# Local attention with a pooled branch and two expert layers: the order of the first two units, of one copy on ACT and of four weight loads

## The chip, the cores and the metric

One core of a Trainium2 chip runs the whole program. The metric is the device time of one execution in microseconds (us). Times inside an execution are counted from the first instruction of the profiled one. ACT is ScalarE, and the SP queue is the queue of loads that SyncE issues.

## What is computed

Per batch and head, attention over 576 positions in two branches that are added: a local one (keys at a distance under 4) and one in which queries, keys and values are averaged by fours, with its output repeated four times. Two layers with a nonlinearity between two products follow.

```
out_d = sm_attn(q_d, k_d, v_d)              # pooled by 4, 144 positions
out_up = np.repeat(out_d, 4, axis=2)
mask = np.abs(pos[:, None] - pos[None, :]) < 4
scores = np.where(mask, scale * q @ k.T, -1e9)
x = out_up + softmax(scores) @ v            # batch 4, heads 8, seq 576, head_dim 64
h = x @ w_in;  g = h * tanh(softplus(h));  x = g @ w_out      # 2304 x 512, d_ff 2048
h = x @ w_in2; s = h * softmax(h); x = layernorm(s) * g_ln @ w_out2   # d_ff 1024
```

## The kernel before

The attention stage works on 16 units (`UNITS`); a unit is one batch and two heads, whose 2 x 64 dimensions fill the 128 partitions. The order on each engine is written out by hand: each engine has one loop over u, and the engines meet at semaphores. Unit u is scored in step u and its output is made in step u + 2 (`LATE`).

What happens to a unit:

- SyncE loads queries and keys into `qkT` (three buffers, L406, L407), windows of V for the local branch into `vw` (four loads, L389), and V in rows of four positions into `v4` (`v` in the profile, L415, L417). Its loop over s issues queries and keys of unit s, windows of unit s - 3 and V of unit s - 2. In steps 14 and 15 it adds the first quarter of the first layer's w_in, two loads of 256 KB in each (`load_w_in(0, kdx)`, L395, into `wraw`). The other quarters and w_out follow behind the loop.
- GpSimd sums queries and keys by four (`pool_queries_keys`, L489, L491; VectorE does the keys of every second unit and both of unit 0, L1079) and the values (`pool_values`, L500, L501), and multiplies the local probabilities with the reciprocal of their sum (`normalise_local`, L508).
- TensorE makes the pooled scores (`score_pooled`, L590), then the local scores in ten windows with a mask added by a matmul (`score_local`, L603, L609). Two steps later it turns both sets of probabilities (`turn_pooled` L624, `turn_local` L633) and multiplies them with the values (`value_pooled` L644, `value_local` L660).
- VectorE takes the maxima of the pooled scores (`maxima_pooled`, L1104, L1107, giving `pbias`), then maximum and subtraction of the local ones (`subtract_local`, L1113, L1116), later the sum of the local exponentials (`sum_local`, L1123) and the reciprocals of all denominators at once (`denominators`, L1130, L1132), which wait for both branches. It copies the local output into `xy` (`evict_local`, L1140).
- ACT takes the exponentials (`exp_pooled` L843, with sums; `exp_local` L874), normalises the pooled probabilities (`normalise_pooled`, L852), copies the turned ones (L864, L869), and copies the pooled output into `od` (`evict_pooled`, L878).

Towards the end of the loops the first layer begins. A float32 weight or activation is split into a high part, rounded to the type that TensorE multiplies fast, and a low part, the rest. ACT makes high parts (`weights_in_high` L885, `split_x` L893), VectorE low ones (`weights_in_low` L1165, `split_x` L1160). `weights_in_high(f)` waits for all four loads of its quarter. On TensorE `hidden(0, 0)` to `hidden(0, 2)` (L674) stand between the last turns and outputs: the first behind the turn of unit 14, the second behind its values, the third behind the turn of unit 15. `turn_pooled(u)` waits for `od_ok` of unit u - 1, that is for `evict_pooled(u - 1)`, since both use one PSUM bank. From there on the first layer runs over 6 blocks of tokens and 16 pieces of d_ff, then the second layer over 18 blocks of tokens.

## Time and profile before

| what | value |
|---|---|
| time, median of 3 runs | 712.12 us (711.85 to 713.67) |
| profiled execution | 710.95 us |
| its span, first to last instruction | 709.2 us |
| busy: TensorE, VectorE, ACT, GpSimd | 679.5, 366.8, 261.1, 184.4 us |
| granted TensorE clock, mean | 0.998 |

The span is 1.75 us shorter than the profiled execution's time, and that time is 1.17 us below the median. GpSimd's 184.4 us lie for the most part in the attention stage. A busy TensorE is not a TensorE at its peak, since matmuls are pipelined.

### The profile page before, as it was taken

The page shows a single profiled execution, that of the slowest core. Times are in us where ns is not written, and L with a number is a line of the kernel's source. Part 1 is how long each engine was busy: PE and PEld are TensorE (multiplying, and loading weights), DVE is VectorE, ACT ScalarE, POOL GpSimd, SP SyncE. Part 2 cuts the span into 40 slices and gives each one's busy share as a digit, 9 for nine tenths or more (in the row PEclk, how much of TensorE's full clock was granted, in tenths as well). Part 3 has the DMA queues.
Part 4 walks back from the last instruction along what each step waited for, and adds up shares of the span by engine and source line. Part 5 has one row for each costly group of instructions (what it writes and reads, how often), then busy time and mean ns, then how long its engine had stood idle before and what let it go on. Part 6 is the DMA issues. An engine that isn't in the chain of part 4 may idle for free.

```text
span 709.2 us, 12611 instructions
## 1 busy us (share of the span) xinstructions
PE 679.5 (96%) x5098; PEld 630.8 (89%) x5098; DVE 366.8 (52%) x675; ACT 261.1 (37%) x583; POOL 184.4 (26%) x221
## 2 busy tenths in 40 slices
PE   5888789999999999999999999999989999999998
PEld 4777679999999999999999999999768888888886
DVE  6999867642233223322232322564796667656671
ACT  3888665332112211221121122135564544444441
POOL 4899830000000000000000000584535434354100
PEclk9999999999999999999999999999999999999999
DMA  6877784000000000000000030002100000000001
GB/s 212 233 228 233 225 275 179 1 0 1 1 1 1 0 1 1 1 1 0 1 1 1 1 118 1 1 1 68 53 16 16 30 31 16 16 31 30 31 16 44
DMA packets 25657, 37.51 MB, mean 53 GB/s; under 512 B 2944, under 2 KB 13184, under 8 KB 25472
## 3 DMA queue, kind: packets, MB, share of 16 engines
q1 hardware_dynamic: 25600, 36.72, 16.2%
q8 instruction: 40, 0.66, 0.4%
q14 instruction: 17, 0.14, 0.1%
HBM read 31.99 MB, written 4.72 MB: 52 GB/s over the span
## 4 chain that ended last, share of the span: by engine, by line
PE 83%; POOL 8%; issue 4%; DVE 3%; DMA 1%; ACT 1%; SPq 0%; POOLq 0%; DVEq 0%
PE psum L674 28%; PE psum L688 28%; PE psum L781 12%; PE psum L758 11%; POOL half_v L500 2%; PE psum L767 2%; POOL half_qk L489 2%; POOL vd L501 1%; POOL prob L508 1%; POOL qd L491 1%; POOL ylo L551 1%; DMA qkT<-kT_dram 1%; DVE so L1304 1%; POOL kd L491 1%; PE psum L660 0%
## 5 line engine op out<-in xcount | busy, mean ns | idle before, releaser
L1201 DVE CAST ghi<-g_sb 128x384 fp32r<-128x384 f32 x96 | 39.7, 414 | 245.2 <-PE psum L688 188.3
L898 ACT ACTIVATE g_sb<-psum 128x384 f32<-128x384 f32 x96 | 47.2, 492 | 292.2 <-PE psum L674 287.9
L674 PE MATMUL psum<-xhi,whi 128*128 128x384 f32 x384 | 129.6, 338 | 0.9 <-ACT g_sb L898 0.7
L674 PE MATMUL psum<-xlo,whi 128*128 128x384 f32 x384 | 129.0, 336 | 0.0
L674 PE MATMUL psum<-xhi,wlo 128*128 128x384 f32 x384 | 129.0, 336 | 0.0
L688 PE MATMUL psum<-ghi,wlo 128*128 128x384 f32 x384 | 129.0, 336 | 0.0
L688 PE MATMUL psum<-ghi,whi 128*128 128x384 f32 x384 | 129.0, 336 | 0.0
L688 PE MATMUL psum<-glo,whi 128*128 128x384 f32 x384 | 129.0, 336 | 0.0
L523 POOL TENSOR_TENSOR t<-raw 128x1024 f32<-128x1024 f32 x1 | 2.6, 2637 | 351.0 <-PE psum L688 351.0
L674 PEld LDWEIGHTS psum<-xhi,whi 128*128 128x128 f32 x384 | 72.2, 188 | 1.7 <-ACT g_sb L898 1.2
L688 PEld LDWEIGHTS psum<-ghi,whi 128*128 128x128 f32 x384 | 72.2, 188 | 0.1
L688 PEld LDWEIGHTS psum<-glo,whi 128*128 128x128 f32 x384 | 72.2, 188 | 0.1
L674 PEld LDWEIGHTS psum<-xlo,whi 128*128 128x128 f32 x384 | 72.2, 188 | 0.0
L674 PEld LDWEIGHTS psum<-xhi,wlo 128*128 128x128 f32 x384 | 72.2, 188 | 0.0
L688 PEld LDWEIGHTS psum<-ghi,wlo 128*128 128x128 f32 x384 | 72.2, 188 | 0.0
L1205 DVE TENSOR_TENSOR glo<-g_sb,ghi 128x384 fp32r<-128x384 f32 x96 | 63.3, 660 | 3.3
L781 PE MATMUL psum<-whi,llo 128*128 128x512 f32 x144 | 57.2, 397 | 0.0
L781 PE MATMUL psum<-whi,lhi 128*128 128x512 f32 x144 | 56.7, 394 | 0.0
L781 PE MATMUL psum<-wlo,lhi 128*128 128x512 f32 x144 | 56.1, 390 | 0.0
L758 PE MATMUL psum<-whi,yhi 128*128 128x512 f32 x126 | 51.0, 405 | 2.3 <-POOL ylo L551 1.2
L758 PE MATMUL psum<-wlo,yhi 128*128 128x512 f32 x126 | 49.5, 393 | 0.0
L758 PE MATMUL psum<-whi,ylo 128*128 128x512 f32 x126 | 49.4, 392 | 0.0
(124 smaller groups left out, 1068.1 us busy)
## 6 DMA issues: line engine op xcount, KB each, us to landing
wraw<-w_dram SPq DMA_DIRECT2D x12, 512.0 KB, 7.9
qkT<-qT_dram SPq DMA_DIRECT2D x16, 288.0 KB, 3.5
qkT<-kT_dram SPq DMA_DIRECT2D x16, 288.0 KB, 4.5
out_dram<-ob SPq DMA_DIRECT2D x18, 256.0 KB, 2.0
v<-v_dram SPq DMA_DIRECT2D x16, 256.0 KB, 3.0
vw<-v_dram SPq DMA_DIRECT2D x32, 128.0 KB, 3.3
wraw<-w_dram SPq DMA_DIRECT2D x16, 256.0 KB, 6.0
raw<-w_dram SPq DMA_DIRECT2D x1, 2048.0 KB, 7.2
```

The costliest lines, as they stand in the source:

```text
L489: own(nc.gpsimd.tensor_tensor(halves[:, 0:n], four[:, 0:n, :, 0:2], four[:, 0:n, :, 2:4], ALU.add))
L491: nc.gpsimd.tensor_tensor(dst[:, par, 0:POOLED], halves[:, a, :, 0], halves[:, a, :, 1], ALU.add).then_inc((pool_q, pool_k[0])[a], 1)
L500: own(nc.gpsimd.tensor_tensor(half_v[:], src[:, :, 0:2 * P], src[:, :, 2 * P:4 * P], ALU.add))
L501: nc.gpsimd.tensor_tensor(vd[:, par, :, :], half_v[:, :, 0:P], half_v[:, :, P:2 * P], ALU.add)\
L674: ins = nc.tensor.matmul(bank, a[:, w], b[:, kdx, :], start=(kdx == 0 and n == 0), stop=(kdx == KD - 1 and n == 2))
L688: ins = nc.tensor.matmul(psum[:, YB + m, 0:N1], a[:, w], b[:, f % GR, :], start=(f == 0 and n == 0), stop=(f == F1 - 1 and n == 2))
L758: ins = nc.tensor.matmul(bank, a[p % 2][:, n, k, :], b[:, w], start=(k == 0 and m == 0), stop=(k == KH - 1 and m == 2))
L767: ins = nc.tensor.transpose(psum[:, T2B + c // 4, (c % 4) * P:(c % 4 + 1) * P], so[:, par, c * P:(c + 1) * P], ident[:])
L781: ins = nc.tensor.matmul(bank, a[:, par, c, :], b[:, w], start=(c == 0 and n == 0), stop=(c == F2 - 1 and n == 2))
L898: nc.scalar.activation(g_sb[:, f % HR, :], psum[:, HB1 + f % HB, 0:N1], ACT.Mish).then_inc(g_ok, 1)
L1201: nc.vector.tensor_copy(ghi[:, f % GR, :], g_sb[:, f % HR, :]).then_inc(ghi_ok, 1)
L1205: nc.vector.tensor_tensor(glo[:, f % GR, :], g_sb[:, f % HR, :], ghi[:, f % GR, :].bitcast(F32), ALU.subtract).then_inc(glo_ok, 1)
```

## The change

Three things are moved; no instruction is added or removed.

- Units 0 and 1 (`FIRST = 2`): TensorE makes the local scores before the pooled ones, VectorE subtracts the local maxima before it takes the pooled ones, and ACT takes the local exponential before the pooled ones.
- In ACT's step 15 the copy of unit 13's pooled output (`evict_pooled`) comes before the pooled exponentials of unit 15, the split of x and the cast of w_in's second piece, and no longer behind them.
- The four loads of w_in's first quarter are issued singly at the ends of steps 8 to 11, and no longer in pairs at the ends of steps 14 and 15.

```diff
+        FIRST = 2
...
+        W_IN = (8, 9, 10, 11)
...
-                if UNITS - 2 <= s < UNITS:
-                    for kdx in range(2 * (s - UNITS + 2), 2 * (s - UNITS + 3)):
-                        load_w_in(0, kdx)
+                if s in W_IN:
+                    load_w_in(0, W_IN.index(s))
...
                 if u < UNITS:
-                    score_pooled(u)
+                    if u >= FIRST:
+                        score_pooled(u)
                     score_local(u)
+                    if u < FIRST:
+                        score_pooled(u)
...
-                if u < UNITS:
+                if FIRST <= u < UNITS - 1:
                     exp_pooled(u)
+                if u >= LATE:
+                    evict_pooled(u - LATE)
                 if u == UNITS - 1:
+                    exp_pooled(u)
                     split_x(0, KD - 1)
                     weights_in_high(1)
-                if u >= LATE:
-                    evict_pooled(u - LATE)
                 if u < UNITS:
                     exp_local(u)
+                if u < FIRST:
+                    exp_pooled(u)
...
                 if u < UNITS:
-                    maxima_pooled(u)
+                    if u >= FIRST:
+                        maxima_pooled(u)
                     subtract_local(u)
+                    if u < FIRST:
+                        maxima_pooled(u)
```

VectorE at the start of the program, from the pooling of unit 0's queries and keys on, before:

```order
L1079 TENSOR_REDUCE qd<-qkT 128x144
L1079 TENSOR_REDUCE kd<-qkT 128x144
L1104 TENSOR_REDUCE psum<-psum 128x3
L1107 TENSOR_SCALAR pbias<-psum 128x3
L1113 TENSOR_REDUCE mx<-psum 128x10
L1116 TENSOR_TENSOR prob<-psum,mx 128x2x5x64
L1079 TENSOR_REDUCE kd<-qkT 128x144
L1123 TENSOR_REDUCE den<-prob 128x10
```

and now (line numbers of the changed kernel):

```order
L1087 TENSOR_REDUCE qd<-qkT 128x144
L1087 TENSOR_REDUCE kd<-qkT 128x144
L1121 TENSOR_REDUCE mx<-psum 128x10
L1124 TENSOR_TENSOR prob<-psum,mx 128x2x5x64
L1112 TENSOR_REDUCE psum<-psum 128x3
L1115 TENSOR_SCALAR pbias<-psum 128x3
L1087 TENSOR_REDUCE kd<-qkT 128x144
L1131 TENSOR_REDUCE den<-prob 128x10
```

The two instructions on the local scores (`mx`, `prob`) have changed places with the two on the pooled ones (`pbias`); TensorE and ACT swap in the same way.

ACT from the turned probabilities of unit 13 to the local exponential of unit 15, before:

```order
L864 COPY pprobT<-psum 128x576
L869 COPY probT<-psum 128x640
L852 ACTIVATE pprob<-pprob,rden 128x144 x3
L843 ACTIVATE pprob,den<-psum,pbias 128x144 x3
L893 CAST xhi<-xy 128x384
L885 CAST whi<-wraw 128x4x128
L878 ACTIVATE od<-psum 128x144
L874 ACTIVATE prob<-prob 128x640
```

and now:

```order
L869 COPY pprobT<-psum 128x576
L874 COPY probT<-psum 128x640
L857 ACTIVATE pprob<-pprob,rden 128x144 x3
L883 ACTIVATE od<-psum 128x144
L848 ACTIVATE pprob,den<-psum,pbias 128x144 x3
L898 CAST xhi<-xy 128x384
L890 CAST whi<-wraw 128x4x128
L879 ACTIVATE prob<-prob 128x640
```

The copy into `od` has moved ahead of five instructions: three exponentials and two casts.

The SP queue now, from V of unit 6 at the end of step 8 to the first load of step 10 and its neighbour (before, no load into `wraw` stood here):

```order
L420 DMA v_57<-v_dram 16x512
L398 DMA wraw<-w_dram 128x512
L409 DMA qkT<-qT_dram 128x576
L410 DMA qkT<-kT_dram 128x576
L392 DMA vw<-v_dram 64x128
L392 DMA vw<-v_dram 64x4x128 x2
L392 DMA vw<-v_dram 64x128
L418 DMA v_57<-v_dram 128x512
L420 DMA v_57<-v_dram 16x512
L398 DMA wraw<-w_dram 128x512
L409 DMA qkT<-qT_dram 128x576
```

One load into `wraw` stands behind V at the end of each of four steps, ahead of queries, keys and windows of the next.

## Rows read from the trace of the kernel before

**Rows 1.** Page, section 2: TensorE's busy tenths in 40 slices of the span.

```profile
PE   5888789999999999999999999999989999999998
```

**Rows 2.** Timeline, start: start us, us, engine, line, operation, count [idle before <-releaser].

```profile
4.26 0.75 DVE L1079 TENSOR_REDUCE qd<-qkT 128x144 f32<-128x576 f32 x1 [0.47 <-DMA qkT<-kT_dram]
...
5.82 1.23 PE L590 MATMUL psum<-kd,qd 64*64 64x144 f32 x8 [5.82 <-DVE kd L1079]
...
8.48 0.38 ACT L843 ACTIVATE pprob<-psum,pbias 128x144 f32<-128x144 f32 x1 [6.46 <-DVE pbias L1107]
...
8.93 0.82 DVE L1113 TENSOR_REDUCE mx<-psum 128x10 f32<-128x640 f32 x1 [0.56 <-PE psum L609]
...
10.65 0.74 ACT L874 ACTIVATE prob<-prob 128x640 f32<-128x640 f32 x1 [0.97 <-DVE prob L1116]
...
12.49 0.24 DVE L1132 RECIPROCAL rden<-dsum 128x13 f32<-128x13 f32 x1
...
12.81 1.26 POOL L508 TENSOR_TENSOR prob<-prob,rden 128x640 f32<-128x640 f32 x1 [4.59 <-DVE rden L1132]
...
18.36 1.26 POOL L508 TENSOR_TENSOR prob<-prob,rden 128x640 f32<-128x640 f32 x1 [0.26 <-DVE rden L1132]
```

**Rows 3.** Timeline of the SP queue, 0 to 125 us: start, time of the issue.

```profile
14.48 1.01 SPq L406 DMA_DIRECT2D qkT<-qT_dram  x1
...
68.47 0.37 SPq L406 DMA_DIRECT2D qkT<-qT_dram  x1
...
73.95 0.90 SPq L395 DMA_DIRECT2D wraw<-w_dram  x2
```

**Rows 4.** Tile vw, last window load of units 11 and 12: issue and landing.

```profile
L389 SPq DMA_DIRECT2D vw<-v_dram x1: 677/677/677, 71.2 to 71.2; - x1
...
DMA to landing us min/median/max: 3.5/3.5/3.5
...
L389 SPq DMA_DIRECT2D vw<-v_dram x1: 1361/1361/1361, 77.7 to 77.7; - x1
...
DMA to landing us min/median/max: 5.6/5.6/5.6
```

**Rows 5.** Timeline, unit 11 to the first hidden matmuls of the first layer.

```profile
75.48 1.26 POOL L508 TENSOR_TENSOR prob<-prob,rden 128x640 f32<-128x640 f32 x1 [0.71 <-DVE rden L1132]
...
75.62 0.80 PE L660 MATMUL psum<-probT,vw 64*64 64x58 f32 x40
...
83.41 0.80 PE L660 MATMUL psum<-probT,vw 64*64 64x58 f32 x40 [1.77 <-issue]
...
86.15 0.62 ACT L885 CAST whi<-wraw 128x512 fp32r<-128x512 f32 x1 [2.88 <-DMA wraw<-w_dram]
...
89.74 0.38 ACT L843 ACTIVATE pprob<-psum,pbias 128x144 f32<-128x144 f32 x1 [0.92 <-DVE pbias L1107]
...
91.37 0.56 DVE L1160 TENSOR_TENSOR xlo<-xy,xhi 128x384 fp32r<-128x384 f32 x1
...
91.74 0.30 ACT L878 ACTIVATE od<-psum 128x144 f32<-128x144 f32 x1
...
92.15 0.77 PE L624 MATMUL psum<-ident,pprob 112*128 112x112 f32 x6 [2.07 <-issue]
...
93.22 0.42 PE L674 MATMUL psum<-xhi,whi 128*128 128x384 f32 x1
...
94.55 1.36 DVE L1165 TENSOR_TENSOR wlo<-wraw,whi 128x512 fp32r<-128x512 f32 x1
...
96.86 0.45 PE L674 MATMUL psum<-xhi,whi 128*128 128x384 f32 x1
```

**Rows 6.** Windows: stretch, busy us by engine, granted clock, DMA share, GB/s.

```profile
30.00:74.00 44.00, 37.36 (x975) 32.30 (x969) 41.15 (x76) 35.90 (x112) 41.17 (x49) 1.00 0.78 226
...
74.50:79.50 5.00, 3.60 (x103) 3.05 (x96) 4.68 (x10) 3.31 (x12) 4.22 (x6) 1.00 0.96 293
...
84.86:88.27 3.41, 3.41 (x50) 3.02 (x50) 3.34 (x7) 2.12 (x5) 2.49 (x3) 0.50 0.66 193
```

## The prediction

> **What bounds the kernel now.** I read the page first: TensorE is busy 679.5 of 709.2 us, and of the 40 slices, 17.7 us each, all under nine tenths are the first six, but for two eights much later [rows 1]. Behind the attention stage the matmuls run nearly back to back, the change does not touch them, and whatever the attention gains or loses moves that block as a whole. So the question is when the attention stage and its hand-over to the first expert layer (0 to about 107 us) end. From here I name units 0 to 15.
>
> In the timeline of the start [rows 2] one unit has the chip to itself. The keys have landed at 4.26. VectorE pools queries and keys, TensorE starts at 5.82 with the pooled scores and ends the local ones just before 8.93, where VectorE's maximum had waited for them. ACT has exponentiated the pooled scores from 8.48, while the local ones reach it at 10.65. The reciprocals come at 12.49, and GpSimd, idle for 4.59 us, normalises unit 0 at 12.81. In between, the long local branch (maximum, subtraction, exponential, sum) waited behind the short pooled one.
>
> From there to unit 12 GpSimd normalises a unit every 5.19 us: (75.48 - 18.36) / 11 [rows 2, 5]. The load queue issues a unit's loads every 5.40 us: (68.47 - 14.48) / 10 [rows 3]. It is slightly slower than the work that it feeds, and its margin melts: the last V-window load of unit 11 lands at 71.2 + 3.5 = 74.7, 0.9 us before TensorE uses it at 75.62. For unit 12, behind the first two quarter loads of w_in (73.95), it lands at 77.7 + 5.6 = 83.3 [rows 3 to 5]. TensorE stood idle for it for 1.77 us, from 81.64 to the use at 83.41 [rows 5].
>
> At the end of the stage [rows 5] there are two more gaps. ACT waits 2.88 us for w_in's four pieces before its cast at 86.15. TensorE waits 2.07 us at 92.15 for the copy of the pooled output of unit 13 (91.74), which ACT holds behind the pooled exponentials of unit 15 (89.74), a split and a cast. Last, the windows view: TensorE has the granted clock 0.50 from 84.86 to 88.27, the 1.2 GHz level, right after the gap at 81.64, and is fully busy there [rows 6].
>
> **Part 1, local scores first in units 0 and 1.** TensorE needs only the raw loads for the local scores, so it starts at about 4.35 and is done by 6.4 (some 2.1 us: the 3.1 from 5.82 to 8.93 less what the pooled scores have alone). The pooled scores then end at about 8.0. VectorE's maximum and subtraction take 1.7 us (8.93 to 10.65 before), so the local exponential starts at 8.2, not 10.65. The pooled maxima (under 1 us: the pooled scores end near 7.5, the exponentials start at 8.48) follow at 8.2 to 9.0, and the pooled exponentials (three of 0.38 with their sums, some 1.2 us) end at 10.3. The local sum is ready by 10.5 behind the keys' reduction of unit 1. Both denominators wait for the later one, and the reciprocals come at about 10.8 instead of 12.49. GpSimd normalises unit 0 at 11.0: a gain of 1.8. Its next work until 18.10 is serial, so it is free at 16.3 and finds the reciprocals of unit 1 ready, for which it had waited 0.26 us [rows 2]; in unit 2 it is much the same. I put the gain of the compute side at 2.3 us, between 1.8 and 2.5. The price is that unit 1's pooled scores wait for unit 0's later pooled exponentials (10.3); behind that wait stand only the turns of unit 0, which need GpSimd's 11.0 + 1.26 anyway. The load queue gains less: it waits for both scores of units 0 and 1, and its loads of unit 4 go out at about 12.5, when those of unit 3 are issued, against 14.48 [rows 3]: 2.0 us.
>
> **Part 2, w_in's first quarter.** The four loads leave the steps of units 14 and 15 and stand singly in four consecutive steps, 8 to 11. Every later load is behind them, on the SP queue and on the DMA engines. Without w_in, unit 12's windows would land one period after unit 11's, at 74.7 + 5.4 = 80.1; with two quarter loads ahead they landed at 83.3, so these cost 1.6 us each there. That is the upper bound. The lower one is the issue alone, 0.90 / 2 = 0.45 us [rows 3]. For the size between: the DMA engines carried 226 GB/s at a share of 0.78 without w_in and 293 GB/s at 0.96 with it [rows 6], so they take more when more is queued, and a quarter of 0.26 MB at 293 GB/s is 0.9. Spread out, with some of the idle share to fill, I take 0.8. Unit 12's windows then land at 80.1 - 2.0 + 4 x 0.8 = 81.3. The compute side would want them at 81.64 - 2.3 = 79.3, so the load decides, and TensorE is 83.41 - 81.3 = **2.1 us** earlier. The waits are then spread over units 9 to 12; what they delay on TensorE is the next turn and scores, on VectorE the copy of the local output and the sum behind it.
>
> The row says that these queues have little room: share 0.78, and two extra loads came through as a stall. The Trainium skill, DMA: Bandwidth & Descriptors (Specifications), gives 512 B as the smallest transfer at line rate and about 358 GB/s for a core's HBM side; by that, an estimate, a unit and a quarter of w_in (1.5 MB) need 4.1 us of the 5.2 and the loads would be free. No stretch of the attention here shows such a rate.
>
> **Part 3, unit 13's pooled output first.** Its input is ready when TensorE ends it, near 89.3, while the pooled exponentials wait for VectorE until 89.74. So the copy fits in the gap, costs 0.3 us of ACT and delays nothing. The turn of unit 14 then starts when TensorE ends its work at 90.1 (92.15 - 2.07). The first hidden matmuls start when VectorE's split is done, at 91.95 (91.37 + 0.56), instead of 93.22; and the second group waits for the low half of w_in's second piece, done at 95.91 (94.55 + 1.36), instead of 96.86 [rows 5]. Gain on the path: **0.95 us**, not 2.07. What is late next is that split and that piece.
>
> **What parts 2 and 3 give together at the hand-over.** With w_in long landed, the 2.88 us wait of ACT goes, and copies, splits and casts behind it come earlier. Without a gap like that at 81.64 the clock stays at 2.4 GHz, which is worth up to 3.41 / 2 = 1.7 us of TensorE [rows 6]. But VectorE's low halves come serially and take over: I count 0.55 us beyond the 0.95, between 0 (clock dips again) and 1.1. So from unit 12's local values to the second hidden group: **1.5 us**.
>
> Sum: 2.1 + 1.5 = 3.6 us, a span of 705.6 against 709.2. The profiled execution was 710.95, 1.2 under the median of the runs, 712.12. The change is applied to the median: 712.12 - 3.6 = **708.5 us**. The first layer's later loads are issued earlier too, and TensorE's slices from the seventh on show no place where they are late now [rows 1].
>
> **Rivals.** (a) The w_in loads are free in the middle. Then the compute side decides: TensorE at 79.3, gain 4.1, and 1.6 at the hand-over: 706.4. For it: the idle DMA share; landing margins of some 2 us around unit 9. Against: the queue is slower than the work that it feeds [rows 2, 3, 5], and the margin is 0.9 by unit 11 with nothing added. The Trainium skill's rule above would have it so. (b) They cost 1.2 each, near what two in a row cost. Unit 12's windows land at 82.9, gain 0.5, and 1.4 behind it: 1.9, 710.2. Then the head start is mostly eaten, since a stage bound by its loads gains only what the queue gained. (c) Slower: with 1.6 each the windows land at 80.1 - 2.0 + 6.4 = 84.5, 1.1 us later than now; four gaps instead of one each lower the clock for a stretch as at 84.86, of which I charge one more at 1.6 us, and the hand-over keeps its own dip and gains nothing: + 2.7, 714.8. It decides from 1.45 us per load, where 78.1 + 4 x 1.45 - 83.4 + 1.6 comes to 2.1. Against it: here one load comes per unit, with a unit's time to drain. (d) Part 1 does not do what it says, because the pooled branch becomes the long one: the reciprocals would come at 12.0 and the gain would be 0.7 there; with the rest, 709.8.
>
> **How the numbers follow.** A measurement of this kernel can tell about 0.3%, 2.1 us, from no change; faster means under 710.0. My forecast (load cost 0.5 to 1.0 each, gains 2.6 to 4.8) has a chance of 0.50; (a) 0.20; (b) 0.16; (c) 0.06; (d) 0.08, half of it beyond the line. Faster: 0.50 + 0.20 + 0.04 + a quarter of (b), 0.04 = 0.78; slower 0.06; the rest, 0.16, is the same. The range goes from (a), 706.4, past (b) to 711.0; it leaves out (c) and the far ends of (a) and (b).
>
> **What would show it.** Right: GpSimd's first normalisation near 11.0; unit 4's queries issued near 12.5; the last window load of unit 12 landed near 81.3; no ACT wait for w_in; no granted clock under 1.0 in the stage; the turn of unit 14 without a wait for the pooled output; the matmuls of the first layer starting some 3.6 us earlier. Wrong: waits of TensorE on windows in units 9 to 12 of over 3 us in sum, or a half clock there (b, c); none at all (a); a first normalisation at 12 (d).

## The result, and the profile after

| | before | after |
|---|---|---|
| median | 711.85 us (709.31 to 713.67, 9 runs) | 708.51 us (707.27 to 710.03, 9 runs) |
| profiled execution, its span | 710.95, 709.2 us | 708.51, 706.7 us |
| granted TensorE clock, mean | 0.998 | 1.0 |

The ratio is 0.9957, with an interval of 0.994 to 0.9973: faster by 3.1 us of 712, between 1.9 and 4.3. The profiled executions differ by 2.5 us in span. The forecast was 708.5, within a range of 706.4 to 711.0.

The page of the changed kernel, its span and TensorE's slices; compare [rows 1]:

```profile
span 706.7 us, 12612 instructions
...
PE   6887889999999999999999999999989999999998
```

Three of the first six slices have changed (the first, fourth and fifth), each by a tenth, and none behind them. TensorE's busy time is 679.5 us, as before. The last 599 us, from 107 us on here and from 109.5 us on before, hold 593.2 us of TensorE's work in both: the block behind the attention only moved.

The timeline of the start (start, length, engine, line, operation, count, and in brackets the idle time before it and its releaser), against [rows 2]:

```profile
4.61 0.48 PE L605 MATMUL psum<-maskb,identb 64*64 64x320 bf16 x4 [4.61 <-DMA qkT<-kT_dram]
...
6.22 0.82 DVE L1121 TENSOR_REDUCE mx<-psum 128x10 f32<-128x640 f32 x1 [0.31 <-PE psum L611]
...
8.00 0.74 ACT L879 ACTIVATE prob<-prob 128x640 f32<-128x640 f32 x1 [5.99 <-DVE prob L1124]
...
8.66 0.38 ACT L848 ACTIVATE pprob<-psum,pbias 128x144 f32<-128x144 f32 x1
...
10.58 1.26 POOL L510 TENSOR_TENSOR prob<-prob,rden 128x640 f32<-128x640 f32 x1 [2.40 <-DVE rden L1140]
...
15.82 1.26 POOL L510 TENSOR_TENSOR prob<-prob,rden 128x640 f32<-128x640 f32 x1
```

TensorE starts 1.2 us earlier, at 4.61 and not 5.82. The local maximum is at 6.22 (before 8.93), the local exponential at 8.00 (10.65), the pooled exponentials now come behind it (8.66), and GpSimd normalises unit 0 at 10.58 (12.81) and unit 1 at 15.82 (18.36).

The SP queue: queries of units 4 and 8, the first of the four loads into `wraw`, queries of unit 12, against [rows 3]:

```profile
12.86 0.37 SPq L409 DMA_DIRECT2D qkT<-qT_dram  x1
...
32.82 1.35 SPq L409 DMA_DIRECT2D qkT<-qT_dram  x1
...
39.05 0.42 SPq L398 DMA_DIRECT2D wraw<-w_dram  x1
...
57.60 0.38 SPq L409 DMA_DIRECT2D qkT<-qT_dram  x1
```

Unit 4's queries go out 1.62 us earlier than the 14.48 of before. From unit 8 to unit 12, where the four new loads stand, the queue takes 24.78 us, 6.19 a unit, against 5.21 before. Unit 12's queries are then issued at 57.60, 0.4 us later than the 57.17 of before: the queue's head start is gone.

The groups of waits from 40 to 90 us (engine, tile, line, what it waited for: us in all, times, longest):

```profile
PE psum L662 <- issue: 5.5, 5, 1.3
...
POOL half_v L502 <- DMA v<-v_dram: 1.1, 1, 1.1
```

TensorE waits five times for windows of V (L662 multiplies them), once in each of the units 8 to 12, 5.5 us in sum. Before there was one such wait, the 1.77 us of unit 12 [rows 5]. Not all of it is added time: the waits ahead of the turns (L626, L624 before) fell from 4.5 to 2.3 us in the same stretch. GpSimd waits once for V too.

The timeline from unit 12 to the first hidden matmuls, against [rows 5]:

```profile
75.09 1.26 POOL L510 TENSOR_TENSOR prob<-prob,rden 128x640 f32<-128x640 f32 x1 [1.71 <-DVE rden L1140]
...
82.06 0.80 PE L662 MATMUL psum<-probT,vw 64*64 64x58 f32 x40 [0.81 <-issue]
...
82.94 0.60 ACT L890 CAST whi<-wraw 128x512 fp32r<-128x512 f32 x1
...
85.89 1.74 DVE L1173 TENSOR_TENSOR wlo<-wraw,whi 128x512 fp32r<-128x512 f32 x1
...
86.82 0.29 ACT L883 ACTIVATE od<-psum 128x144 f32<-128x144 f32 x1 [0.20 <-PE psum L646]
...
88.25 0.77 PE L626 MATMUL psum<-ident,pprob 112*128 112x112 f32 x6 [0.76 <-issue]
...
88.39 0.38 ACT L848 ACTIVATE pprob<-psum,pbias 128x144 f32<-128x144 f32 x1 [1.28 <-DVE pbias L1115]
...
90.00 0.45 PE L676 MATMUL psum<-xhi,whi 128*128 128x384 f32 x1 [0.43 <-DVE prob L1124]
...
94.42 0.44 PE L676 MATMUL psum<-xhi,whi 128*128 128x384 f32 x1 [0.38 <-DVE wlo L1173]
```

The story of the stage can be read from GpSimd's normalisations, since there is one per unit:

| unit | 0 | 2 | 4 | 6 | 8 | 9 | 10 | 11 | 12 |
|---|---|---|---|---|---|---|---|---|---|
| before | 12.81 | 23.16 | 34.15 | 43.83 | 54.81 | 60.06 | 64.49 | 70.15 | 75.48 |
| after | 10.58 | 20.25 | 31.23 | 40.90 | 51.88 | 57.13 | 62.73 | 68.93 | 75.09 |
| earlier by | 2.2 | 2.9 | 2.9 | 2.9 | 2.9 | 2.9 | 1.8 | 1.2 | 0.4 |

The head start made in units 0 and 1 is carried to unit 9 and then melts to 0.4 within three units, those whose windows stand behind the new loads. Unit 12's local values start at 82.06, 1.35 earlier. Between these and the second group of hidden matmuls, at the hand-over, another 1.09 us comes: that group starts at 94.42 and not at 96.86, 2.44 earlier, and the span is 2.5 shorter. ACT's cast of w_in (82.94) has no wait, the turn of unit 14 (88.25) one of 0.76 and not 2.07.

### The profile page after: what moved, and what is told of

It is laid out like the page before. It is cut to its first block, busy times and chain, and to the rows that moved or that the text cites. A ratio compares the mean times of both kernels' runs of the same rounds, so it can differ in the third digit from the quotient of the medians.

```text
span 706.7 us, 12612 instructions
## 1 busy us (share of the span) xinstructions
PE 679.5 (96%) x5098; PEld 629.5 (89%) x5098; DVE 366.6 (52%) x675; ACT 261.2 (37%) x583; POOL 183.7 (26%) x221
## 4 chain that ended last, share of the span: by engine, by line
PE 84%; POOL 6%; DVE 4%; issue 3%; ACT 1%; DMA 1%; SPq 0%; POOLq 0%; DVEq 0%; ACTq 0%
PE psum L690 28%; PE psum L676 28%; PE psum L786 12%; PE psum L763 11%; PE psum L772 2%; POOL half_v L502 2%; POOL half_qk L491 1%; POOL prob L510 1%; POOL ylo L553 1%; PE psum L662 1%; DMA qkT<-kT_dram 1%; POOL vd L503 1%; POOL qd L493 1%; PE psum L646 1%; DVE so L1315 1%
```

## The experiments

Each run has one profiled execution, and executions of one kernel differ: the two profiles of the changed kernel have spans of 706.7 and 708.2 us. So a profile is read here for the order of events, and the times for sizes. Where the profiled execution was the fastest or slowest of its run, this is said.

My theory after the result: part 1 and part 3 gain, part 2 costs nearly a microsecond a load, because the loads take the place of others in the SP queue or on the DMA engines. The rivals: part 2 gains at the hand-over what it costs in the middle; part 3 gives nothing by itself; and the cost is the bytes, so that it would be the same from any queue.

### Each part alone, and parts 1 and 3 together

**e1_part1**, part 1 alone:

```diff
-                if s in W_IN:
-                    load_w_in(0, W_IN.index(s))
+                if UNITS - 2 <= s < UNITS:
+                    for kdx in range(2 * (s - UNITS + 2), 2 * (s - UNITS + 3)):
+                        load_w_in(0, kdx)
...
-                if FIRST <= u < UNITS - 1:
+                if FIRST <= u < UNITS:
                     exp_pooled(u)
-                if u >= LATE:
-                    evict_pooled(u - LATE)
                 if u == UNITS - 1:
-                    exp_pooled(u)
                     split_x(0, KD - 1)
                     weights_in_high(1)
+                if u >= LATE:
+                    evict_pooled(u - LATE)
```

> Part 1 alone; w_in's first quarter and the copy of unit 13's pooled output stand as before. Theory (the middle of the stage is bound by its loads): GpSimd normalises units 2 to 11 some 2.9 us earlier, as with the whole change, but from unit 12 on the loads decide, which started 1.6 to 2.2 us earlier; TensorE uses unit 12's windows near 81.2 (83.4 before) and the time falls by 2.2 us, between 1.6 and 2.6. Rival A (bound by the engines): the full 2.9 reaches the end. Rival B (the head start is lost to the slower load queue even without the moved loads): under 1 us.

Measured: ratio 0.9979 (0.9962 to 0.9995), 1.5 us faster. TensorE at unit 12 and at the turn of unit 14, and a window (stretch, busy us of TensorE, its weight loads, VectorE, ACT and GpSimd, granted clock, DMA share, GB/s):

```profile
81.15 0.80 PE L663 MATMUL psum<-probT,vw 64*64 64x58 f32 x40 [2.63 <-issue]
...
89.93 1.35 PE L627 MATMUL psum<-ident,pprob 112*128 112x112 f32 x6 [3.35 <-ACT od L884]
...
89.80:93.20 3.40, 3.27 (x15) 3.15 (x16) 2.63 (x5) 1.48 (x4) 1.31 (x2) 0.50 0.91 261
```

Unit 12's local values start at 81.15, 2.26 us earlier than before, as expected of it (near 81.2). The forecast of the whole change had 2.1 there, with w_in's cost in it. But only 1.5 us is left in the times. TensorE then waits 3.35 us for the pooled output of unit 13, where the kernel before waited 2.07, and behind that wait the clock is 0.50, its 1.2 GHz level, with the engine nearly fully busy: from 89.80 to 93.20 that costs up to 1.7 us. The profile before had a half clock too, at 84.86 [rows 6], so that between these two profiles it is mostly the longer wait that takes the gain back.

**e2_part2**, part 2 alone: `FIRST = 0`, and ACT's step 15 as before.

```diff
-        FIRST = 2
+        FIRST = 0
```

> Part 2 alone: the four loads in steps 8 to 11, scores and copy as before. Theory (each load in the middle costs what the queue and the DMA engines take for it, about 0.6 us): GpSimd's normalisations slip in units 10 to 12 by over 1 us, TensorE uses unit 12's windows at 84.0 or later, and the gain at the hand-over (no wait of ACT for w_in) about pays for that: 0.5 us slower, between 0.3 faster and 1.3 slower. Rival (the loads fit into idle time in the middle, and two in a row near the end were the bad place): 1 to 2 us faster.

Measured: ratio 1.0027 (1.0016 to 1.0038), 1.9 us slower: less than the 0.3% that I call telling, but the interval lies above 1 as a whole. TensorE's first and last group of unit 12's windows, the turn of unit 14, and a window, in the slowest of the nine executions:

```profile
83.39 0.68 PE L662 MATMUL psum<-probT,vw 64*64 64x58 f32 x30
...
85.08 0.43 PE L662 MATMUL psum<-probT,vw 64*64 64x58 f32 x10 [1.00 <-issue]
...
93.74 1.38 PE L626 MATMUL psum<-ident,pprob 112*128 112x112 f32 x6 [3.62 <-issue]
...
92.60:99.40 6.80, 5.66 (x22) 5.51 (x23) 3.69 (x6) 3.50 (x9) 3.68 (x3) 0.50 0.83 264
```

GpSimd normalises unit 12 at 77.31, 1.8 us later than before, as expected (over 1 us). But unit 12's first windows are multiplied at 83.39, just when they were before (83.41), where 84.0 or later was expected; the last ones follow at 85.08. The pieces of w_in are there early, and nothing comes of it: TensorE stands for 3.62 us at the turn of unit 14 for the pooled output, and runs at half clock for 6.80 us. The second hidden group starts at 101.13, so that all the 4.3 us by which this span is longer (713.5 and 709.2) lie behind unit 12's first windows. Part 2 buys nothing by itself; how much of its loss is the loads' own cost, and how much the longer wait and the clock that part 3 takes away, this run does not tell.

**e3_part3**, part 3 alone: `FIRST = 0`, and the four loads as before.

> Part 3 alone: the copy of unit 13's pooled output first. Theory: the turn of unit 14 starts near 90.1, the second hidden group near 95.9 instead of 96.86, 0.95 us faster in the trace. Rival: the whole gap of 2.07 us comes back. Second rival: nothing, since ACT's later work (the exponentials of unit 15) is pushed back and decides.

Measured: ratio 0.9962 (0.995 to 0.9974), 2.7 us faster, no half clock in its profile. That is nearly three times the forecast 0.95, and more than the whole gap of 2.07 that it removes [rows 5]. In the profile 1.4 us of it lies ahead of the part: the windows of unit 12 happened to be used at 82.0. From unit 12's local values to the second hidden group it takes 12.4 us here, 13.45 before and 15.0 in e1_part1. So against the profile before, part 3 is worth 1.1 us on the path, near the forecast, and against one like that of e1_part1, with its longer wait and a half clock behind it, 2.7.

The granted clock of all executions, and not of the profiled ones alone, tells which of the two is common. Its mean over an execution was 1.0 in four of the five of this run, and 0.997 in the fifth. Of the 17 executions of the kernel before that ran beside it, none had over 0.999 and the mean was 0.996. The profile of the kernel before, with its one half clock and 0.998, was thus one of the better ones. The difference of 0.0036 in the mean clock is up to 2.6 us of TensorE's time in 712 (an estimate), which covers what the path alone leaves open. Where in an execution the clock was lost the means do not say.

**e4_parts13**, parts 1 and 3, the four loads as before:

```diff
-                if s in W_IN:
-                    load_w_in(0, W_IN.index(s))
+                if UNITS - 2 <= s < UNITS:
+                    for kdx in range(2 * (s - UNITS + 2), 2 * (s - UNITS + 3)):
+                        load_w_in(0, kdx)
```

> Parts 1 and 3 without part 2. Theory: 2.2 + 0.95 = 3.1 us faster, so as fast as the whole change (3.3 by the medians, 2.5 by the traces) or slightly faster: part 2 is worth nothing once part 1 is there, since its four loads take 2.5 us of the head start between units 9 and 12 and give 1 to 2 back at the hand-over. Rival: part 2 is worth 1 us or more, then this one is 2.3 us faster than before or less.

Measured: ratio 0.9943 (0.993 to 0.9957), 4.1 us faster, by the ratios 0.5 to 1.0 us more than the change itself (0.995 and 0.9957), and just what e1_part1 and e3_part3 add up to (1.5 + 2.7). TensorE at unit 12 and at the turn of unit 14:

```profile
81.20 0.80 PE L663 MATMUL psum<-probT,vw 64*64 64x58 f32 x40 [2.17 <-issue]
...
87.40 0.77 PE L627 MATMUL psum<-ident,pprob 112*128 112x112 f32 x6 [0.76 <-issue]
```

Both stand 0.85 us earlier than in the changed kernel (82.06, 88.25), although unit 12 waits 2.17 us for its windows. So the change is likely better without its part 2. The intervals of the two ratios overlap (0.993 to 0.9957 and 0.994 to 0.9973), so that this is not shown by the times of this run alone; e2_part2, where part 2 alone is slower, says the same.

### What part 2 pays for

**e5_w_start**, all three parts, with the four loads at the end of step 2, issued near 4.6 us:

```diff
-                if s in W_IN:
-                    load_w_in(0, W_IN.index(s))
+                if s == 2:
+                    for kdx in range(KD):
+                        load_w_in(0, kdx)
```

> The whole change, but with the four loads of w_in's first quarter issued together behind V of unit 0 at about 4.6 us, where the SP queue then waits for the first scores until 7.9. Theory (loads in the middle cost about 0.6 us each, and here they fall into an idle stretch): normalisations keep some 2.9 us up to unit 11, no or a small wait for windows in units 8 to 12, unit 12's local values at 79.3 to 80.5, hand-over 1.1 to 1.5 better than before: 4.5 us faster than before, between 3.6 and 5.6, and 1 to 2.5 faster than the change. Rival (the head start is lost anyway, because the load queue is slower than the engines): as fast as the change. Second rival: the loads delay V of unit 0 and the queries of unit 3, and the start loses 1 us or more.

Measured: ratio 0.9937 (0.9915 to 0.996), 4.5 us faster, as forecast. The times scatter (705.4 to 710.7), so against the change that ran beside it (3.6 faster) this is likely and no more. In its profile TensorE waits once for windows from 40 to 90 us, 1.4 us in unit 11, and unit 12's local values start at 78.8, earlier than expected (79.3 to 80.5). The loads cost little there, where the queue issues nothing else until 7.66.

**e6_eight**, the dose: w_in's second quarter too is issued in steps 8 to 11, eight loads instead of four.

```diff
                 if s in W_IN:
                     load_w_in(0, W_IN.index(s))
+                    load_w_in(1, W_IN.index(s))
...
-            for kdx in range(KD):
-                load_w_in(1, kdx)
```

> The whole change, with the second quarter of w_in also loaded in steps 8 to 11: two loads per step, eight in the middle, and four fewer behind the stage. Theory: each further load costs another 0.6 us or more, TensorE uses unit 12's windows at 84.4 or later (82.06 with the change) and the time is 2 to 4 us over the change. Rival (the engines have room, the delay with four was only jitter): within 1 us of the change.

Measured: ratio 0.9985 (0.997 to 1.0), 2.6 us above the change by the medians of e8_change_again and this kernel, which shared their chip (708.80 and 711.39): 0.65 us per added load. The profiled execution (708.14 us) was the fastest of the twelve and does not show this cost. In it unit 12's local values start at 81.58, and not at 84.4 or later as expected, and the queue takes 6.35 us a unit from unit 8 to unit 12, little more than with four loads (6.19); it has a half clock from 60.4 to 63.8. Part of the 2.6 us may be the clock: its mean over all executions was 0.996 here and 0.999 in e8_change_again.

**e7_act_queue**, the four loads from ACT's queue, in ACT's steps 6 to 9; the SP queue has none in the attention:

```diff
-        W_IN = (8, 9, 10, 11)
+        W_IN_ACT = (6, 7, 8, 9)
...
-                if s in W_IN:
-                    load_w_in(0, W_IN.index(s))
...
+            def load_w_in(c, kdx):
+                at = kdx * FF1 + c * WQ
+                src = w1_d[2 * kdx + c // 2][:, c % 2 * WQ:(c % 2 + 1) * WQ]
+                act.dma_start(wraw[:, at:at + WQ], src).then_inc(ld_wi[c], 16)
...
+                if u in W_IN_ACT:
+                    load_w_in(0, W_IN_ACT.index(u))
```

> The whole change, with the same four loads at about the same times (39 to 55 us), but issued from ACT's queue behind the local exponentials of units 6 to 9, so that they take no issue time of SyncE. If the cost of the loads in the middle is SyncE's issue time (0.47 us each), normalisations keep 2 us or more at unit 12 and the time is 1.5 us under the change. If it is the DMA engines' time, it is within 0.6 us of the change, on either side. If ACT's own issue time counts, it is slower.

Measured: ratio 0.9927 (0.9913 to 0.994), 706.53 us (705.31 to 708.42), **the fastest kernel of the study** by its median: 5.2 us under the kernel before by the ratio, and 2.3 under the change that ran beside it by the medians, with intervals of the ratios that just overlap (0.9913 to 0.994 and 0.9937 to 0.9963). From e5_w_start it can't be told apart. The profiled execution (705.31) was the fastest of the six. GpSimd's normalisation of unit 12, TensorE's local values of it, the turn of unit 14, and the window that has the four loads in it; under them the same window of the changed kernel:

```profile
72.64 1.26 POOL L508 TENSOR_TENSOR prob<-prob,rden 128x640 f32<-128x640 f32 x1 [0.71 <-DVE rden L1145]
...
78.73 0.80 PE L660 MATMUL psum<-probT,vw 64*64 64x58 f32 x40
...
85.21 0.77 PE L624 MATMUL psum<-ident,pprob 112*128 112x112 f32 x6 [1.03 <-issue]
...
40.00:58.00 18.00, 15.57 (x409) 13.26 (x409) 16.41 (x33) 15.11 (x48) 16.82 (x19) 1.00 1.01 283
```

```profile
40.00:58.00 18.00, 15.25 (x409) 13.09 (x404) 16.51 (x33) 15.11 (x48) 16.75 (x20) 1.00 0.88 250
```

The bytes are the same and are asked for at about the same time (38.1 to 53.9 us). TensorE waits for no window in units 8 to 13, and unit 12 starts 3.3 us before the change's. The DMA engines move 283 GB/s at a share of 1.01 and not 250 at 0.88. So they had room for w_in; the SP queue had little. From unit 8 to unit 12 it takes 5.21 us a unit here, and 5.05 of these are spent in issues (33 loads); it waits for no semaphore there. With the four loads of the change it is 5.87 of 6.19. e11_act_no3 and e12_act_no1, which have the loads on ACT's queue too, do have waits for windows, 2.2 and 1.5 us: none at all is what the best execution shows.

**e8_change_again**, the changed kernel once more, beside e5 to e7 (no edit):

> The changed kernel unaltered, as the yardstick for the three beside it: 3.3 us faster than before (2.3 to 4.3). In its trace the waits of TensorE for windows should again stand in units 8 to 12 and add up to 4 to 6 us; the half clock of the kernel before should be absent, or be present only behind such a wait.

Measured: ratio 0.995 (0.9937 to 0.9963), 3.6 us faster, in agreement with 0.9957. The waits for windows are 5.6 us in four, as expected. In its profiled execution (span 708.2, the slowest of five) unit 12's local values start at 83.3 and there is a half clock in the middle, right behind a wait of 1.68 us for windows:

```profile
71.30:74.70 3.40, 3.40 (x51) 2.92 (x51) 2.14 (x4) 0.87 (x3) 2.08 (x3) 0.50 0.79 215
```

Rival (c)'s price is thus paid in some executions of the changed kernel, though not in the one shown first.

**e9_tiny**, e7_act_queue with four dummy loads of 4 KB (128 rows of `g_ln`, 32 B each) on the SP queue, where the change has its loads of 256 KB:

```diff
+                if 8 <= s < 12:
+                    sp.dma_start(tiny[:, 8 * (s - 8):8 * (s - 7)], gln_d).then_inc(ld_tiny, 16)
...
+            sp.wait_ge(ld_tiny, 64)
```

> The kernel with w_in's four loads on ACT's queue, and in their old places on the SP queue, at the ends of steps 8 to 11, four dummy loads of the same 128 rows but only 4 KB each (g_ln into a spare tile): SyncE's issue time and place in the queue without the bytes. If what the loads cost on the SP queue is its issue time (0.4 to 0.5 us each, about 1.8 in all), the waits for windows in units 8 to 12 come back in part and the time is 1 to 2.5 us above the kernel without the dummies (706.5). If it is the bytes in the SP queue's ring, within 0.6 us of that kernel.

Measured: ratio 0.9949 (0.9934 to 0.9965), 1.6 us above e7_act_queue by the ratios, whose intervals just overlap; the two ran on different chips. The profiled execution (711.86) was the slowest of the twelve, and that of e7_act_queue the fastest of its six, so that the differences between the two profiles are larger than those of the kernels. The SP queue (the second dummy load, and an issue of queries), GpSimd's normalisation of unit 12, and the window:

```profile
45.60 0.41 SPq L425 DMA_DIRECT2D tiny<-gln_dram  x1
...
53.21 1.92 SPq L411 DMA_DIRECT2D qkT<-qT_dram  x1
```

```profile
76.82 1.26 POOL L513 TENSOR_TENSOR prob<-prob,rden 128x640 f32<-128x640 f32 x1 [1.71 <-DVE rden L1150]
```

```profile
40.00:58.00 18.00, 14.40 (x395) 12.59 (x397) 15.46 (x31) 14.06 (x43) 15.49 (x19) 1.00 0.78 236
```

Sixteen kilobytes in all cost most of what a megabyte did (1.6 us, and 2.3 from e7_act_queue to the change). Unit 12 is normalised 4.2 us later than in e7_act_queue, and at 76.82 even later than in the change (75.09). The queue takes 6.32 us a unit from unit 8 to unit 12, of which 6.15 are issues, and 5.21 without the dummies, of which 5.05 are. The share of the DMA engines falls to 0.78. This profile has a half clock near 81.6 to 85 us besides. A load's own issue takes 0.41 us; the rest shows in longer issues of other loads (1.92 us at 53.21, where most take 0.37), though single issues of over a microsecond stand in e7_act_queue too (1.43 us at 48.73). So the evidence is for the load as such and not its size. What in it stays open: a dummy has 128 rows like a load of w_in, so that slots of a queue that fill by rows would look the same as time of issue, and no run tests whether rows of 32 B are handled more slowly than their bytes alone would ask.

**e10_act_late**, e7_act_queue with the four loads in pairs behind ACT's steps 12 and 13:

```diff
-        W_IN_ACT = (6, 7, 8, 9)
+        W_IN_ACT = (12, 13)
...
-                    load_w_in(0, W_IN_ACT.index(u))
+                    for kdx in range(2):
+                        load_w_in(0, 2 * W_IN_ACT.index(u) + kdx)
```

> The four loads on ACT's queue again, but in pairs behind the local exponentials of units 12 and 13, at about 72 and 78 us, where the kernel before had them on the SP queue. If the queue matters and not the place, it is as fast as with steps 6 to 9 (706.5, within 0.6 us). If the place matters (two loads in a row make unit 12's windows late, or the cast waits for w_in), it is 1 us or more slower, and ACT shows a wait for w_in again.

Measured: ratio 0.9959 (0.9938 to 0.998), 709.92 us, but between 706.4 and 714.4. Its profile (span 707.6) has 4.4 us of waits for windows in units 9 to 11, and a half clock behind the last of them (77.5 to 80.9). From unit 8 to unit 12 its queue takes 5.77 us a unit, as in e8_change_again, although no load of w_in is issued there. ACT waits for no piece of w_in. This run is inconclusive: such scatter is the stage's own, and it hides what the later place costs. It also warns of the table below: a period or a sum of waits from one profile proves little.

### Parts 1 and 3 on the better kernel

**e11_act_no3** and **e12_act_no1**, e7_act_queue without part 3 and without part 1:

```diff
-                if FIRST <= u < UNITS - 1:
+                if FIRST <= u < UNITS:
                     exp_pooled(u)
-                if u >= LATE:
-                    evict_pooled(u - LATE)
                 if u == UNITS - 1:
-                    exp_pooled(u)
                     split_x(0, KD - 1)
                     weights_in_high(1)
+                if u >= LATE:
+                    evict_pooled(u - LATE)
```

```diff
-        FIRST = 2
+        FIRST = 0
```

> Parts 1 and 2 with the loads on ACT's queue, without part 3: no wait for windows is left in the stage, so that the gap ahead of the turn of unit 14 stands alone. By my count on the path part 3 is worth 0.95 us. By the three traces without part 3, each with a half clock near this hand-over, and the medians of part 3 alone (3 us), it is worth 2 to 3: 708.5 to 709.5, with a granted clock of 0.5 right behind the gap in this trace or a large spread of its times.

> Parts 2 and 3 with the loads on ACT's queue, without part 1: what the first two units' order is worth when the load queue takes nothing back. In the traces the head start was 2.9 us at unit 2; if all of it reaches the end, 2.9 us slower than with part 1, 709.4. Alone on the old kernel part 1 gave 1.5 by the medians; if it is worth only that here too, then something else than the loads takes the rest: 708.

Measured: e11_act_no3 0.9961 (0.9947 to 0.9975), 2.4 us above e7_act_queue, with intervals apart: part 3 is worth here what it was worth alone. The turn of unit 14 and the window behind it:

```profile
90.16 1.26 PE L624 MATMUL psum<-ident,pprob 112*128 112x112 f32 x6 [3.30 <-issue]
...
90.30:93.70 3.40, 3.40 (x16) 3.25 (x16) 2.91 (x5) 1.56 (x4) 1.59 (x2) 0.50 0.87 265
```

A wait of 3.30 us, and a half clock right behind it, as expected. Not as expected, there was a wait for windows as well, 2.16 us in unit 11, with a half clock of its own near 77 to 80 us. The mean clock over all executions was 0.995, and 0.999 in e7_act_queue. From unit 12's local values to the second hidden group it takes 15.3 us, against 12.5 in e7_act_queue. e12_act_no1 gave 0.9949 (0.9929 to 0.9969): part 1 is worth 1.6 us there (4.0 by the spans of the two profiles, 707.5 and 703.5), with overlapping intervals. That is less than the 2.2 to 2.9 us by which it brings the units forward.

### The parts in one table

The last two columns are the granted clock, mean of all executions of the run, and the SP queue's period from unit 8 to unit 12 in the one profile.

| kernel | part 1 | w_in's first quarter | part 3 | ratio to before | us of 712 | clock | queue, us a unit |
|---|---|---|---|---|---|---|---|
| before | no | SP, steps 14, 15 | no | 1 | 0 | 0.9957 | 5.21 |
| e1_part1 | yes | as before | no | 0.9979 | -1.5 | 0.9956 | 5.18 |
| e2_part2 | no | SP, steps 8 to 11 | no | 1.0027 | +1.9 | 0.9951 | 5.84 |
| e3_part3 | no | as before | yes | 0.9962 | -2.7 | 0.9994 | 5.44 |
| e4_parts13 | yes | as before | yes | 0.9943 | -4.1 | 0.9985 | 5.26 |
| the change (again) | yes | SP, steps 8 to 11 | yes | 0.9957 (0.995) | -3.1 (-3.6) | 0.9992 (0.9990) | 6.19 (5.77) |
| e5_w_start | yes | SP, step 2 | yes | 0.9937 | -4.5 | 0.9988 | 5.19 |
| e6_eight | yes | SP, steps 8 to 11, and the second quarter | yes | 0.9985 | -1.1 | 0.9964 | 6.35 |
| e7_act_queue | yes | ACT, steps 6 to 9 | yes | 0.9927 | -5.2 | 0.9993 | 5.21 |
| e9_tiny | yes | ACT, steps 6 to 9; SP: four dummies | yes | 0.9949 | -3.6 | 0.9980 | 6.32 |
| e10_act_late | yes | ACT, steps 12, 13 | yes | 0.9959 | -2.9 | 0.9965 | 5.77 |
| e11_act_no3 | yes | ACT, steps 6 to 9 | no | 0.9961 | -2.8 | 0.9953 | 5.32 |
| e12_act_no1 | no | ACT, steps 6 to 9 | yes | 0.9949 | -3.6 | 0.9983 | 5.50 |

In the four profiles with four additional loads on the SP queue in this stretch its period is 5.77 to 6.32 us, with eight 6.35, and in the nine others 5.18 to 5.77: a load adds to it, but profiles of one kind differ by as much as half a microsecond. The clock falls in two places: without part 3 at the turn of unit 14, and in the middle of the stage, mostly behind waits for windows.

The three parts alone come to -2.3 (-1.5 + 1.9 - 2.7), the change to -3.1 or -3.6: part 2 costs less in the company of part 3 than alone.

## Why the prediction was right, and where only its sum was

The time was forecast as 708.5 and measured as 708.51. That is closer than its steps were, and the last 0.3 us of it is luck: I took 3.6 us from a median of 712.12, and the gain was 3.3 us from a median of 711.85. Among the steps the gain of part 3 was put too low, and the cost of part 2 too.

**Part 1.** Right in mechanism, and as an event in the trace: first normalisation 10.58 (forecast 11.0), so rival (d), which had it at 12.0, is out. The head start of the compute side is 2.9 us from unit 2 to unit 9, beyond my upper bound of 2.5; of unit 0 itself it is 2.2. The queue gained less than forecast: unit 4's queries at 12.86 (12.5), 1.62 us and not 2.0. In the times part 1 alone is worth 1.5 (interval 0.4 to 2.7).

**Part 2.** This is the step that failed in its reason. I priced a load by its bytes: a quarter of 0.26 MB at 293 GB/s. The price was near: unit 12's windows were used at 82.06, where I had 81.3, and by my own formula, 78.1 + 4 x cost, that is 1.0 per load and not 0.8, or 0.9 with the head start of 1.62 us that the queue really had; by the normalisations it is (2.9 - 0.4) / 4 = 0.63. But e7_act_queue has the same bytes and no cost that its profile shows, and e9_tiny puts nearly no bytes back on the SP queue and has most of the cost. What was short was the SP queue, and the row that says so was in my hands: SyncE issues a unit's loads every 5.40 us, slower than the work they feed [rows 2, 3], while the DMA share was 0.78 [rows 6]. I used the first row for the margin and the second for the price. That the queue itself was short is shown in the times with intervals that just overlap, and in the profiles by a queue that does hardly anything but issue.

The Trainium skill, DMA: Bandwidth & Descriptors (Specifications), gives about 358 GB/s as the limit of a core's HBM side, and by my estimate from it the loads would have been free. From 40 to 58 us the runs reached 250 GB/s with the loads on the SP queue, where they were not free, and 283 with them on ACT's. For about half a microsecond even the kernel before passes 358 (394 GB/s near 49 us), so that my "no stretch" holds for longer ones alone. The same page (Issuing engines are not separate DMA queues) says that issuing from several engines saves only the time on the sequencer, usually small beside the transfer. Here this was no small thing: 2.3 us of the kernel's time by the medians of e8_change_again and e7_act_queue, nearly as much as part 3 is worth.

I had also counted 0.55 of the hand-over's 1.5 us for w_in landed early and the clock. ACT's wait of 2.88 us for w_in did go, as forecast, but e4_parts13 keeps the late loads and takes 12.4 us from unit 12's local values to the second hidden group, just as the change does (12.36), with a wait of ACT of 2.94 us for w_in still in it. So that wait was covered, and in the profile of the change the 0.55 us did not come: the hand-over gained 1.09, and e3_part3 gains the same with part 3 alone. By the ratios part 2 is a loss of 0.5 to 1.0 us on top of the others (4.1 against 3.6 or 3.1), which is within the intervals, and of 1.9 alone.

**Part 3.** Forecast 0.95 us on the path. The order of events was right: the turn of unit 14 no longer waits for `od`, and behind it the split of x and the low half of the second piece decide ("0.38 <-DVE wlo L1173" before 94.42). On the path, between profiles, its size was near too: 1.1 us (13.45 to 12.36, in e3_part3 and in the change). In the times it was not: 2.7 alone, 2.4 on top of e7_act_queue, 2.6 between e1_part1 and e4_parts13. The missing term is the clock. I had charged a half clock to the gap at 81.64 and not to the gap of 2.07 at the turn, because in the profile of before the clock was full there. That profile was not typical: it has a mean clock of 0.998, and the 63 executions of the kernel before that ran beside the experiments average 0.996, with one above 0.998. In e1_part1, e2_part2 and e11_act_no3 the gap is 3.3 to 3.6 us and a half clock follows at once; in the ten profiled executions with part 3 (the change's two among them) the clock is full from 86 us on, through the whole hand-over. One profiled execution showed one of two ways in which this end can go, and the rarer one. Why the clock falls in the one and not in the other was not shown.

**The rivals.** (a), free loads, was refuted for the SP queue, and describes e7_act_queue: I had 706.4, it ran 706.53. Its "for" (the idle DMA share) was right, its place wrong. That the sums meet is in part luck: its steps were 4.1 us at unit 12 and 1.6 behind it, and the profile has 4.7 and 1.0. (b), 1.2 per load and 710.2: too dear, but its remark that a stage bound by its loads gains only what the queue gained is what units 10 to 12 show. (c): its mark, over 3 us of waits for windows in units 9 to 12, is there, 4.4 us and with unit 8 5.5, and its half clock is in e8_change_again. Yet the time is faster, since these waits consumed a head start, and in part took the place of waits ahead of the turns; the mark was badly chosen.

**The sum.** Forecast: 2.1 at unit 12 and 1.5 behind it. Measured in the spans: 1.35 and 1.09, with 2.5 in all. In the medians, -3.3. An execution can differ from another by some 2 us in this stage, so the spans are read for places, and the times for sizes.

## What to carry to other kernels

Ask of a load that is moved which queue it passes, and compare that queue's period with the period of the work that it feeds: here a load on a queue without slack delayed unit 12 by 0.6 to 1.0 us in the profile and the kernel by 0.1 to 0.65 us in its time, and from another queue no cost was seen. A profile is one execution: the granted clocks of all executions say whether it is a typical one. A gap of TensorE costs more than its length where the clock falls behind it, as at the turn of unit 14; such a gap, just ahead of dense work, is worth more than its length on the path. A head start is worth only what the slowest feeder can follow.

## What was not expected of the hardware

- Four loads of 4 KB held the SP queue about as much as four of 256 KB: its period was 6.32 us a unit with the small ones, 6.19 and 5.77 in the two profiles with the large ones, and 5.21 in e7_act_queue with neither. Their own issues take 0.41 and 0.42 us.
- With a few loads a unit the SP queue issued nearly without a pause: 5.05 of 5.21 us in e7_act_queue, 6.15 of 6.32 in e9_tiny.
- The same four loads from ACT's queue, each 0.33 to 0.41 us of issue, raised what the DMA engines moved in the same 18 us from 250 to 283 GB/s.
- After waits of TensorE of 3.30, 3.35 and 3.62 us the granted clock was 0.50 for 3.4 or 6.8 us, right behind them. Shorter waits had it or not: 1.77 us [rows 5, 6] and 1.68 (e8_change_again) had one behind them, and 2.07 [rows 5], 2.17 (e4_parts13) and 2.63 us (e1_part1, at 81.15) had none. What decides it in such a case stays open.
- Whether it is issue time or places in the queue that a load takes was not told apart: a dummy load in one row, and not 128, would do it and was not run.
